# Three interleaved transposes and twelve 64x128 split pieces in the two mixtures of an attention + two-MoE kernel

## What is computed

```
x = _attn_ref(x, weight_gen)      # softmaxed 7-tap weights per token and head, [2, 3584, 192] -> 7168 rows of 192
x = _moe_ref(x, ...)              # top 2 of 8 experts: out += w * (relu(x @ w1[e]) @ w2[e]), F = 1024
x = _moe2_ref(x, ...)             # top 1 of 8 experts by cosine, the same two products with other weights
```

## Time and profile before

| | |
|---|---|
| time, median of 3 runs | 1233.42 us (1232.42 to 1233.71) |
| the profiled execution: its time | 1230.78 us |
| its span, first to last instruction | 1229.0 us |
| mean granted TensorE clock | 0.959 |
| PE busy | 1098.7 us (89%) |
| DVE busy | 753.6 us (61%) |
| ACT busy | 548.3 us (45%) |
| POOL busy | 523.5 us (43%) |

### The profile page before, as it was taken

The page is one execution under the profiler, slowest core; times in us unless marked ns, Lnnn a source line. Parts: engine busy times, 40 slices in busy tenths (PEclk is TensorE's granted clock), DMA queues, the critical chain, the costliest instruction groups (busy, mean ns, idle before and its releaser), DMA issues.

```text
span 1229.0 us, 27241 instructions
## 1 busy us (share of the span) xinstructions
PE 1098.7 (89%) x8062; PEld 1041.1 (85%) x8062; DVE 753.6 (61%) x1412; ACT 548.3 (45%) x1543; POOL 523.5 (43%) x635
## 2 busy tenths in 40 slices
PE   1999168999999999999999999787289999999997
PEld 0566056999999999999999999766279999999997
DVE  8998896546465554646545464476854654466663
ACT  2112266445454544545445454356644554455552
POOL 5878102444444444444444444400324444444444
PEclk9999589999999999999999999989589999999999
DMA  9111200313122131312213111173712313124511
GB/s 330 67 58 65 60 1 21 95 42 95 38 73 67 41 102 42 94 38 79 64 41 97 39 37 38 40 257 104 239 50 72 100 39 102 40 61 128 141 56 36
DMA packets 51188, 97.89 MB, mean 80 GB/s; under 512 B 9651, under 2 KB 33051, under 8 KB 50876
## 3 DMA queue, kind: packets, MB, share of 16 engines
q1 hardware_dynamic: 33084, 61.77, 16.4%
q0 software_dynamic: 18048, 35.42, 9.9%
HBM read 69.62 MB, written 29.10 MB: 80 GB/s over the span
## 4 chain that ended last, share of the span: by engine, by line
PE 78%; DVE 13%; issue 3%; POOL 2%; ACT 2%; DMA 2%; DVEq 0%; POOLq 0%; ACTq 0%; SPq 0%
PE banks L605 22%; PE banks L607 11%; PE banks L591 9%; PE banks L597 7%; PE banks L596 7%; PE banks L592 7%; PE banks L593 7%; DVE prods L856 3%; PE banks L567 2%; POOL prods L415 2%; PE banks L575 2%; PE banks L576 2%; PE banks L529 1%; DVE choices L1064 1%; PE banks L519 1%
## 5 line engine op out<-in xcount | busy, mean ns | idle before, releaser
L1014 DVE SCALAR_TENSOR_TENSOR h_lo<-banks,h_hi 128x256 fp32r<-128x256 f32 x736 | 312.0, 424 | 373.6 <-ACT h_hi L743 319.0
L743 ACT ACTIVATE h_hi<-banks 128x256 fp32r<-128x256 f32 x736 | 282.5, 384 | 450.8 <-PE banks L597 340.1
L605 PE MATMUL banks<-w_hl,h_hi 128*128 128x384 f32 x1472 | 466.4, 353 | 0.0
L607 PE MATMUL banks<-w_hl,h_lo 128*128 128x192 f32 x1472 | 371.1, 252 | 0.0
L607 PEld LDWEIGHTS banks<-w_hl,h_lo 128*128 128x128 f32 x1472 | 279.6, 190 | 0.0
L605 PEld LDWEIGHTS banks<-w_hl,h_hi 128*128 128x128 f32 x1472 | 276.0, 188 | 0.2
L430 POOL DMA_INDIRECT x_slots<-token_rows,gather_idx x192 | 192.3, 1002 | 107.2 <-POOL gather_idx L427 76.8
L591 PE MATMUL banks<-x_hi_a,w_hi 128*128 (+1 forms) x736 | 224.9, 306 | 1.7 <-DVE x_hl_b L982 1.7
L592 PE MATMUL banks<-x_hi_a,w_lo 128*128 (+1 forms) x736 | 206.6, 281 | 0.0
L597 PE MATMUL banks<-x_hl_b,w_lo 128*128 (+1 forms) x736 | 206.3, 280 | 0.0
L596 PE MATMUL banks<-x_hl_b,w_hi 128*128 (+1 forms) x736 | 205.8, 280 | 0.0
(11 more groups left out here) (172 smaller groups left out, 1271.7 us busy)
## 6 DMA issues: line engine op xcount, KB each, us to landing
raw<-in_moe_w SPq DMA_DIRECT2D x17, 768.0 KB
choices<-choice_rows SPq DMA_DIRECT2D x28, 384.0 KB, 3.8
raw<-in_moe_w SPq DMA_DIRECT2D x17, 512.0 KB
raw<-in_moe_w SPq DMA_DIRECT2D x34, 256.0 KB
x_halo<-in_x SPq DMA_DIRECT2D x2, 2688.0 KB, 15.0
token_rows<-stage SPq DMA_DIRECT2D x14, 384.0 KB, 2.3
token_rows<-rows SPq DMA_DIRECT2D x14, 384.0 KB, 3.9
x_slots<-token_rows,gather_idx POOLq DMA_INDIRECT x192
```

What stands on the lines that cost most here:

```text
L605: mm(y[:, i, 0:2 * D], h_hi[:, c % HBUFS, t], w2_hl[u][:, c, :, :], start=c == 0, stop=False)
L607: ins = mm(y[:, i, 0:D], h_lo[:, c % HBUFS, t], w2_hl[u][:, c, 0, :], start=False, stop=c == FC - 1)
L743: sc.activation(h_hi[:, c % HBUFS, :], banks[:, c % HBANKS, 0:BLOCK], ACT.Relu).then_inc(h_hi_ready[m], 1)
L1014: v.scalar_tensor_tensor(h_lo[:, c % HBUFS, :], banks[:, c % HBANKS, 0:BLOCK], 0.0, h_hi[:, c % HBUFS, :].bitcast(F32), ALU.max, ALU.subtr ...
```

## The change

`turn_slots` makes three transposes instead of four. Transpose `i` takes every third feature (`i`, `i + 3`, ...) of both halves at once, 64 features of half 0 on partitions 0 to 63 and the same 64 of half 1 on partitions 64 to 127. The two halves of a third therefore lie on different partitions of bank 3, while the products want them side by side in columns; so `x_hi` and `x_lo` become six 64x128 pieces each (three thirds, two halves), several of which write to other partitions than they read. The rows of `w1` are loaded in the same interleaved order, which takes five DMAs for an expert instead of four, of the same bytes. The turn moves from chunk 2 to chunk 1; the high pieces of half 0 and 1 are made in ACT's chunks 2 and 3, the low pieces in DVE's chunks 4 and 5.

```
-TURN_AT = 2
+TURN_AT = 1
-X_SPLIT_AT = 4
+X_HI_AT = 2
+X_LO_AT = 4
+WEIGHT_LOADS = 16 * 5
...
+        def half_slots(h):
+            return slice(h * P, (h + 1) * P)
+        def rows_of(n):
+            return slice(n * DB, (n + 1) * DB)
+        def turned_half(i, h):
+            return banks[rows_of(h), 3, half_slots(i)]
+        def x_hi_place(hi_a, part_b, i, h):
+            return hi_a[rows_of(i), half_slots(h)] if i < THIRDS - 1 else part_b[rows_of(h), half_slots(h)]
+        def x_lo_place(lo_a, part_b, i, h):
+            return lo_a[rows_of(i), half_slots(h)] if i < THIRDS - 1 else part_b[rows_of(1 - h), half_slots(h)]
...
-                for src, dst in ((wa[e, 0:DA, :], raw1[:, 0, :]),
-                                 (wa[e, DA:D, :], raw1[0:DB, 1, :]),
-                                 (wa[e, DA:D, :], raw1[DB:P, 1, :]),
+                third = lambda r: wa[e].rearrange("(f r) q -> r f q", r=THIRDS)[r]
+                for src, dst in ((third(0), raw1[0:DB, 0, :]),
+                                 (third(1), raw1[DB:P, 0, :]),
+                                 (third(2), raw1[0:DB, 1, :]),
+                                 (third(2), raw1[DB:P, 1, :]),
...
-                    for i in range(HALVES):
-                        nc.tensor.transpose(banks[:, 3, i * P:(i + 1) * P], x_slots[:, i, 0:DA], ident[:])
-                        ins = nc.tensor.transpose(banks[0:DB, 3, BLOCK + i * P:BLOCK + (i + 1) * P], x_slots[:, i, DA:D], ident[:])
+                    thirds_of_halves = x_slots[:].rearrange("p h (f r) -> p r (h f)", r=THIRDS)
+                    for i in range(THIRDS):
+                        ins = nc.tensor.transpose(banks[:, 3, i * P:(i + 1) * P], thirds_of_halves[:, i, :], ident[:])
...
-                    sc.copy(hi_a, banks[:, 3, 0:BLOCK])
-                    sc.copy(part_b[0:DB], banks[0:DB, 3, BLOCK:]).then_inc(x_hi_ready[m], 1)
+                    for i in range(THIRDS):
+                        ins = sc.copy(x_hi_place(hi_a, part_b, i, h), turned_half(i, h))
+                    if h == HALVES - 1:
+                        ins.then_inc(x_hi_ready[m], 1)
...
-                        if c == X_SPLIT_AT:
-                            x_hi(g + 1)
+                        if X_HI_AT <= c < X_HI_AT + HALVES:
+                            x_hi(g + 1, c - X_HI_AT)
...
-                    v.tensor_tensor(lo_a, banks[:, 3, 0:BLOCK], hi_a.bitcast(F32), ALU.subtract)
-                    v.tensor_tensor(part_b[DB:P], banks[0:DB, 3, BLOCK:], part_b[0:DB].bitcast(F32),
-                                    ALU.subtract).then_inc(x_split[m], 1)
+                    for i in range(THIRDS):
+                        ins = v.tensor_tensor(x_lo_place(lo_a, part_b, i, h), turned_half(i, h),
+                                              x_hi_place(hi_a, part_b, i, h).bitcast(F32), ALU.subtract)
+                    if h == HALVES - 1:
+                        ins.then_inc(x_split[m], 1)
...
-                        if c == X_SPLIT_AT:
-                            x_lo(g + 1)
+                        if X_LO_AT <= c < X_LO_AT + HALVES:
+                            x_lo(g + 1, c - X_LO_AT)
```

More of the change, by code:

```diff
@@ L372, in _ @@
             load_expert(v1, v2, 0)
-            sp.wait_ge(raw_in, 64 * (2 * E + 1))
+            sp.wait_ge(raw_in, WEIGHT_LOADS * (2 * E + 1))
         @block.gpsimd
@@ L415, in _ @@
                     gp.tensor_tensor(taps[:, to], taps[:, to], taps[:, other], ALU.add).then_inc(taps_added, 1)
-            pool.wait_ge(raw_in, 64)
+            pool.wait_ge(raw_in, WEIGHT_LOADS)
             gp.tensor_copy(w1_hi[0][:], raw1[:]).then_inc(pool_step, 1)
@@ L707, in mixture, with x_hi @@
             def mixture(m):
-                def x_hi(g):
+                def x_hi(g, h):
                     hi_a, _, part_b = x_buffers(parity(act, g))
-                    act.wait_ge(x_turned[m], g + 1)
-                    sc.copy(hi_a, banks[:, 3, 0:BLOCK])
-                    sc.copy(part_b[0:DB], banks[0:DB, 3, BLOCK:]).then_inc(x_hi_ready[m], 1)
+                    if h == 0:
+                        act.wait_ge(x_turned[m], g + 1)
+                    for i in range(THIRDS):
+                        ins = sc.copy(x_hi_place(hi_a, part_b, i, h), turned_half(i, h))
+                    if h == HALVES - 1:
+                        ins.then_inc(x_hi_ready[m], 1)
                 act.wait_ge(table_ready[m], 1)
                 ends = expert_ends(act, m)
-                x_hi(0)
+                for h in range(HALVES):
+                    x_hi(0, h)
                 def split_next(u, c, expert):
                     if c == 0:
-                        act.wait_ge(raw_in, expert * 64 + 64 * (E * m + 2))
+                        act.wait_ge(raw_in, expert * WEIGHT_LOADS + WEIGHT_LOADS * (E * m + 2))
                     half = FC // 2
@@ L976, in mixture, with x_lo @@
             def mixture(m):
-                def x_lo(g):
+                def x_lo(g, h):
                     hi_a, lo_a, part_b = x_buffers(parity(dve, g))
-                    dve.wait_ge(x_hi_ready[m], g + 1)
-                    v.tensor_tensor(lo_a, banks[:, 3, 0:BLOCK], hi_a.bitcast(F32), ALU.subtract)
-                    v.tensor_tensor(part_b[DB:P], banks[0:DB, 3, BLOCK:], part_b[0:DB].bitcast(F32),
-                                    ALU.subtract).then_inc(x_split[m], 1)
+                    if h == 0:
+                        dve.wait_ge(x_hi_ready[m], g + 1)
+                    for i in range(THIRDS):
[3 more added lines that the diff above has]
+                        ins.then_inc(x_split[m], 1)
                 dve.sem_inc(y_ready[m], 2)
@@ L988, in mixture @@
                 ends = expert_ends(dve, m)
-                x_lo(0)
+                for h in range(HALVES):
+                    x_lo(0, h)
                 def split_next(u, c, expert):
```

## The result

The changed kernel takes **1298.14 us** (median of 6 runs, 1296.36 to 1300.79), the kernel before in the same job 1232.58 us (6 runs). The ratio is 1.053, with a 95% interval of 1.052 to 1.055. The forecast was slower, 1254.7 us in a range of 1239 to 1272: the direction is right, the size is not, by 43 us.

A forecast was written before the change was run, and what follows sets the result against it. PE was taken to bound the mixtures, with DVE setting PE's start in switch blocks. 1230.8 - 4.6 (plain) + 21.3 (switch) + 4.6 (first blocks) = 1252.1, plus 2.6 to the median: 1254.7 us, range 1239 to 1272.

The forecast's parts named there:

- the plain block: Step for blocks without weight splitting: ACT in time, h_lo(6) ends at 9.38, next block at 9.66 us, cover used up exactly.
- 76 x (9.66 - 9.72) = -4.6: Sum term for the 76 plain blocks: each falls from 9.72 to 9.66 us, saving 4.6 us in all.
- The third rival: Pieces dearer, 0.34 us on DVE: plain blocks 9.84, switch blocks +1.7 each, 1271 us in all; chance 0.15.
- plain turns above 9.75: Sign that the forecast is wrong: plain blocks more than 9.75 us from turn to turn, where 9.63 to 9.7 was expected.
- Switch blocks: Blocks that also split weights: DVE's late h_lo(6) delays PE, next block at 11.40 us; +1.5 each, +21.3 for 14.
- DVE's 0.31 a piece: Cost of each 128-column DVE piece, taken without overlap: 0.31 us, 0.93 for a half; bounds 0.21 and 0.34.
- ACT's pieces: ACT's 128-column copies: 0.28 us where output or input partitions move, 0.14 where not; h_hi(4) in switch blocks some 0.8 late.
- 11 of the 12: Count of steps around DVE's pieces held, by the skill's rule, until all earlier instructions have finished.
- the second rival: ACT's pieces overlap, 0.15 us each: h_hi(4) 0.62 earlier, a switch block costs +0.9, 1245 us in all; chance 0.19.
- the shorter turn: PE's three transposes in place of four: 0.35 us against 0.44, 0.09 less a block, 8.3 us at most over 92.
- First blocks: First block of each mixture: first split not hidden, first product 1.8 us later; +2.3 together, twice, +4.6.
- The turn's place adds nothing: Claim that the turn's move costs no time, since gather, turn and next gather keep their distance of one block.

The follow-up runs named there:

- a2: The changed kernel with the gathers of the loops left out, so later blocks work on stale rows: 1258.95 us.
- a1: The changed kernel with one 128x256 GpSimd memset ahead of the gathers of each block: 1295.36 us, ratio 1.053 to the kernel before.
- h_both: a1 with whole ACT and DVE operations in place of the pieces in switch blocks, whose rows are then in wrong order: 1269.62 us.
- c1: The changed kernel with ACT's pieces one chunk earlier, at chunks 1 and 2, and no memset: 1256.23 us, ratio 1.020 to the kernel before.
- d1: The changed kernel with the last of ACT's six pieces left out in plain blocks, so part of those rows is stale: 1256.65 us.
- b1: The changed kernel with a 128x960 GpSimd memset ahead of each pair of gathers in the loops: 1259.46 us, ratio 1.022 to the kernel before.
- c3: b1 with two of DVE's three pieces of half 1 left out in 14 of 16 switch blocks (rows partly stale): 1248.52 us.
- c4: b1 with two of ACT's three pieces of half 1 left out in 14 of 16 switch blocks (rows partly stale): 1250.84 us.
- a3: The kernel before, four transposes and whole copies kept, with only the turn moved from chunk 2 to chunk 1: 1234.98 us, ratio 1.003.
- d5: The changed kernel with ACT's last piece of half 1 written as two, seven pieces in all: 1260.71 us, ratio 1.024 to the kernel before.

## Why the prediction was wrong, and where it was right

**The step that failed** is the plain block: "h_hi(4) 5.87 (ACT is in time) ... next block 9.66". ACT had its work done in time, and h_hi(4) still started 0.6 late. The forecast gave a signal from PE to ACT no time beyond the usual one. The term "76 x (9.66 - 9.72) = -4.6" measured +39: the 76 intervals sum to 769 us after and 730 before. What the runs show in its place: the signal of the matmul is recorded 0.55 to 0.93 us behind its end in 73 of 74 blocks, in a stretch in which POOL's second gather ends, and DVE's list has no cover for that. Without the gathers (a2, on the chip on which a1 and h_both are late) it goes, and the block takes 9.64. What else it takes is not shown. No rival named it. The third rival has plain blocks above today's for dearer pieces; the pieces are 0.29 to 0.30 a step, so that was not it. The prediction's sign "plain turns above 9.75" did come, but not from dearer pieces.

**What was right.** Where the lateness is absent (c1, d1, b1 and a2), the times lie at 1256 to 1259 us beside the 1254.7 of the forecast. Of its terms:
- Switch blocks: 11.40 forecast, 11.40 measured. Undone alone (h_both) they give back 25.7 us; 16 x 1.5 = 24 is their part of the loss against the kernel before. DVE's 0.31 a piece: 0.305 (c3). ACT's pieces are on the path too (c4, 0.43 where 0.35 was worked out).
- The rule of the Trainium skill ("VectorE: DVE Perf Modes", section "Two Vector instructions with no wait between them"): the trace agrees, with 0.30 from a piece to the next at 0.28 to 0.29 long, and h_lo to the first piece 0.34 where nothing holds it. Held are 7 of the 8 steps into and out of the two halves, not "11 of the 12" as the prediction counts; its sum goes by the steps and is not touched. On ScalarE the pieces follow at 0.26 to 0.28, at 0.26 long, so the overlap that the Trainium skill gives ("ScalarE: Activation LUTs", section "What ACT_TABLE_LOAD costs") is not seen where partitions change, and the second rival falls. It is seen into the last piece of half 1, the one step where they stay the same: 0.165 us, with 0.14 forecast.
- Plain blocks, free of the lateness (a2): 9.64, forecast 9.66. They are 0.08 shorter than before (9.72), and 0.09 was forecast from the shorter turn.
- First blocks: PE waits 2.66 us there, not 0.84 as in the earlier trace rows, in line with the 1.8.
- "The turn's place adds nothing" was a little off: in c1 PE waits 6.3 us in all for gathered rows, in 8 waits, before it was 3.4 in 4. Most of these blocks follow a switch block, while the next weights load. And a3 is slower by 0.3% (0.2 to 0.4).

**Still open.** Why a signal from PE is held back for 0.4 to 0.9 us around the end of the second indirect DMA of a pair, in some runs and not in others. The times of ACT, matmul and gather do not decide it: h_hi(7) is late with ACT idle, and c1 has the same times there without a late signal. Nor does the chip alone: a1 and a3 ran in one job on chip 8, some 60 signals of each fall into the last 0.3 us of a second store with ACT idle, and 56 of 58 are late in a1, 1 of 60 in a3. The changed kernel beside c1 and d5 on one chip would have told the edit from the place. Whether the recording of the semaphores, which misses records in the same runs, takes part is not tested. And whether it is the issue of the DMA on POOL or the transfer behind it was not separated: a2 takes out both.

**No version beats the kernel before.** b1's plain blocks with h_both's switch blocks would be at 1259.5 - 25.7 = 1234 by an estimate, and those whole operations need rows laid out by four transposes.

## What to carry to other kernels

Cover that is "used up exactly" should be priced with what a small delay would then cost times the number of blocks: here none was left in 76 blocks, and a lateness of 0.6 at h_hi(4) went through almost in full, while the kernel before took one of the same size at h_hi(0) for nothing. Splitting whole operations by partition costs DVE and ACT a full operation each, because none overlaps; count them in the stretch that is already at its limit (the switch blocks), not in the mean. When a wait seems to end late, look at when its semaphore was recorded as raised, and at every other wait of that kind in the trace: here h_hi(7) contradicts what h_hi(4) suggests. And run the kernel in question again beside each variant that seems to cure it: here b1, c1, d1 and d5 came out 37 to 42 us faster than the changed kernel, on chips where no kernel had a late signal.

## What was not expected of the hardware

- The signal of a finished matmul can be recorded, and take effect on ScalarE, 0.40 to 0.93 us late, while TensorE goes on without a pause. It did so for 125 of the 148 signals that fell into the last 0.3 us of GpSimd's second indirect DMA of a pair, and for none of the 82 at a first one. In the kernel before it was 53 of 68 at second stores and 2 of 85 at second gathers.
- Runs of nearly the same kernel differ in this altogether: 121 to 132 late signals of 736 in the changed kernel, a1 and h_both, and 0 in all thirteen kernels that were run on four other chips.
- A memset of 0.31 us ahead of an indirect DMA moved the second gather's end by 0.04 us only (a1), one of 0.90 us by 0.40 (b1). GpSimd idles 0.8 us ahead of the first gather anyway, and the short memset takes up part of that.
